# Masked attention and two gated layers on one core: six tiles per pair scaled on ScalarE, the split of q and k in eight operations of 384 columns, another order in the first unit of layer one

## The chip, the core and the metric

One core of one Trainium2 chip. Its engines are TensorE (PE, with its weight loads PEld), VectorE (DVE), ScalarE (ACT) and GpSimd (POOL); SyncE (SP) issues the transfers. Each engine takes its own instructions in order, and semaphores tie them together. The metric is the device time of one launch in microseconds, median of the runs.

## The reference

Everything is fp32. Attention over 2 x 8 heads, 768 positions and 64 dimensions, where a query sees only the keys with the same six-bit sign code:

```python
q_bits = (np.einsum('bhsd,dk->bhsk', q, proj) > 0)      # k alike
mask = q_bucket[:, :, :, None] == k_bucket[:, :, None, :]
scores = np.where(mask, scale * np.matmul(q, k.transpose(0, 1, 3, 2)), -1e9)
attn = np.exp(scores - np.max(scores, axis=-1, keepdims=True))
attn = attn / (np.sum(attn, axis=-1, keepdims=True) + 1e-09)
x = np.matmul(attn, v)                                  # heads side by side: 1536 x 512
x = (((x @ w1) * (x @ w2)) @ w3) @ w_out                # d_ff 1024
y = (1 / (1 + np.exp(-(x @ w_gate))) * (x @ w_val)) @ w_out2   # d_ff 1536
```

## The kernel before, in words

TensorE works on fp32r operands, so each fp32 operand is split in a rounded high part and a lower part (the difference), and a product is three matmuls (high x high, high x low, low x high). The splits are the work of the other engines: a rounding (a copy or an add of zero into an fp32r tile) and a subtraction.

**Attention.** Eight pairs of heads, `pair(p)` on each engine; PE runs pair 0, a loop over pairs 1 to 6, and pair 7. A pair has `STEPS` = 12 tiles of 128 queries, tiles 0 to 5 of the first head and 6 to 11 of the second. `UQ` = 3 tiles make a half of a head. For tile k the engines do, each in its own fixed order:

- PE (`pair`, L1271): at k = 1 the code bits of the next pair; `scores` of tile k+2 (four matmuls, L1197; they wait for the exp of tile k); a third of `values` of the half before (four matmuls, L1224); for k >= 4 one piece of `fill`, the product of w3 and w_out (three matmuls, L1257 to L1259); `transpose` of tile k (six, L1209). The transposes wait for the scaled tile (`norm_done`) and, bank by bank, for `pt_lo` of tile k-1.
- DVE (`pair`): `row_max` of tile k+1 (L924), `sum_eps`, `exp_scale`, `inverse` and `exp_bias` (four small ones; `sum_eps` and `inverse` are of tile k and wait for its exp, the other two are of tile k+1), `normalise` of tile k (L949, `prob` times `rnorm`, 128x768) unless ScalarE does it, then `transposed_lo` of tile k-1 (L957, two subtractions into `pt_lo`, each after its half of `pt_hi`), and `code` at k = 2.
- ACT (`pair`): at k = 0 a copy of the `fill` bank (`wp`); at k = 1, 4, 7, 10 the two copies of `attention_halves`; `transposed_hi` of tile k-1 (L617, two copies into `pt_hi`); the scaling of tile k where `k % UQ in NORM_ON_ACT` (L693; it waits for DVE's `rnorm`); then `exp` of tile k+1 (L650, with the sum along the row). Pair 0 also rounds wo1 after k = 3, 4, 6, 7; pair 6 (`ahead`) rounds the first weights of layer one after k = 8 and k = 9 (`pair_raw_high`, `pair_sums_high`); pair 7 (`last`) rounds a first-layer operand after each of k = 9, 10, 11 (`x_operand_high`).
- POOL (`pair`): `attention_sum(p, 0)`, which waits for ACT's halves at k = 1; `w3_split(1)`; `qk_split(p + 1)`, the high and lower part of the next pair's q and k, one instruction each over 1536 columns (L432 and L450, tile `hl`); `scale_q_codes`; `attention_sum(p, 1)`; `v_split` of one head (L432, L458, 384 columns each); `w3_split(0)`; `v_split` of the other head. In a middle pair the `qk_split` lies beside tiles 3 and 4. Pair 6 adds T3's sums and the first weight sums; pair 7 has no `qk_split`, but the sums T2 and T1 (`x_sum`, four of 768 columns), the split of B11 and the rounding of T3.
- SP: per pair two loads of w3 and v, the load of q and k of pair p+2 (after `hl_ready`), and `assemble` for each head, nine copies from `hl`, `codes` and `q_codes` into `sq` and `mk`. `assemble(0)` waits for `hl_ready`, `q_codes_done` and the scores of tile 5; PE's first scores of the next pair wait for it.

**Layer one** follows in units of seven products (a Strassen-like scheme over blocks of x: B11, T3, T2, T1, B22, B21, T4), each on two sides, six matmuls a side (L1296 to L1298). T3 is B22 less the block of pairs 0 and 1, T2 = T3 + B11, T1 = B22 - T2 and T4 = B21 - T2 are sums of blocks. PE's `unit(0, 0)` starts while attention ends: after B11 come the last three parts of `values`, then T3, T2, T1, B22, B21, T4. T2 waits for `u1_kept`, T1 for `u2_kept`, B22 for `u4_kept`: ScalarE's copies of the running bank (`kept1`, `kept2`, `kept4`), which stand in ACT's written-out order among the roundings `x_operand_high` of the operands. The lower parts `x_operand_low` are DVE's, in place over the raw block (L976), in the order `X_LOW_ORDER`. The lower part of T2 overwrites T2, which T4 = B21 - T2 still needs (`x_sum4`, L984), and B21 holds the output of pair 7; so T2's lower part on a side waits for `attention_out` (L963) of that side. B11's split and T3's rounding are POOL's, ahead of time. Then POOL makes the weight sums and lower parts of the next unit (`pair_weights`); PE's next unit waits for `g_ready`. Units run on to the end of layer one, then layer two and three in the same way.

## Time and profile before

| | us |
|---|---|
| median of 3 runs | 776.63 (776.06 to 777.81) |
| the profiled execution, its own time | 775.34 |
| its span | 773.3 |
| busy PE / PEld | 731.5 / 675.3 |
| busy DVE / ACT / POOL | 480.9 / 456.2 / 345.2 |
| granted TensorE clock, mean | 0.995 of full |

About 2.0 us of the profiled execution lie outside its span. Busy times are sums over an engine's instructions; an instruction that waits for something after it has started counts as busy for that time too. A timeline row has the start and length in us, engine, line, operation, what it writes and reads, the number of instructions merged in it, and in brackets the idle time before it with what ended it. A group row has the busy time of the group and the mean ns of one instruction. A middle pair lasts from 135.77 to 171.30 in the rows below, measured from `pt_lo` of tile 2 to the same of the next pair: in it tile 3's transposes are at 136.37, tile 4's at 140.13 and tile 10's at 157.21. The rows of tile 0 to tile 3 late in that window (161 to 171 us) belong to the next pair; what is at 170.06 there was at about 134.53 in the pair before.

### The profile page before, as it was taken

Reading aid. Unit: us, or ns where it says so; the run is one execution under the profiler, and the core shown is the slowest. Engines: PE = TensorE matmul, PEld = TensorE weight load, DVE = VectorE, ACT = ScalarE, POOL = GpSimd, SP = SyncE. Lnnn points to the kernel's source line nnn. Section 1 sums busy time; section 2 is a strip of 40 time slices with the busy share of each in tenths; the row PEclk is TensorE's granted clock in tenths of the full one; section 3 lists DMA queues with packets and bytes.
Section 4 is the critical chain, followed back from the end, with each engine's and each line's share of the span. In section 5 each row is a group of like instructions: output and inputs, shape, how many; then the busy total and the mean of one; then the engine's idle time right before and its main releaser. Section 6 shows DMA issues by size and latency. Waiting matters only on the chain.

```text
span 773.3 us, 12684 instructions
## 1 busy us (share of the span) xinstructions
PE 731.5 (95%) x4136; PEld 675.3 (87%) x4136; DVE 480.9 (62%) x1032; ACT 456.2 (59%) x842; POOL 345.2 (45%) x253
## 2 busy tenths in 40 slices
PE   6798989899898989799999999999999999999998
PEld 4687878778797878799999999999999999988886
DVE  5899999999999999832432833624324326774100
ACT  5788888897888988545446424564454454715100
POOL 3867364554628697164466600054653554140000
PEclk9999999999999999999999999999999999999999
DMA  5774443436273500001001000010010010401001
GB/s 154 219 175 105 116 124 94 129 89 165 71 175 91 115 12 18 28 28 56 28 27 54 1 0 1 1 55 28 28 54 28 27 55 0 163 1 68 28 28 41
DMA packets 26609, 51.79 MB, mean 67 GB/s; under 512 B 4161, under 2 KB 12689, under 8 KB 26577
## 3 DMA queue, kind: packets, MB, share of 16 engines
q1 hardware_dynamic: 26272, 51.32, 24.4%
q8 instruction: 17, 0.28, 0.1%
q14 instruction: 16, 0.12, 0.0%
q10 hardware_dynamic: 304, 0.07, 0.0%
HBM read 29.43 MB, written 3.15 MB: 42 GB/s over the span
## 4 chain that ended last, share of the span: by engine, by line
PE 74%; DVE 13%; issue 6%; ACT 4%; DMA 2%; SPq 1%; DVEq 0%; ACTq 0%
PE pair_bank L1296 14%; PE pair_bank L1298 14%; PE pair_bank L1297 13%; PE bank L1296 5%; PE bank L1298 5%; PE bank L1297 5%; PE bank L1224 5%; PE bank L1209 5%; PE pair_bank L1197 4%; DVE pt_lo L957 4%; DVE rowmax L924 4%; ACT pt_hi L617 2%; DMA qk_raw<-in_qk 2%; DVE prob L949 1%; PE bank L1258 1%
## 5 line engine op out<-in xcount | busy, mean ns | idle before, releaser
L1062 DVE TENSOR_TENSOR u<-bank,u 128x384 f32<-128x384 f32 x80 | 44.3, 555 | 135.5 <-ACT u L617 126.6
L617 ACT ACTIVATE u<-pair_bank 128x384 f32<-128x384 f32 x120 | 58.7, 491 | 109.3 <-PE pair_bank L1298 109.1
L1209 PEld LDWEIGHTS bank<-ident,prob 128*128 128x128 f32 x576 | 65.8, 141 | 49.7 <-DVE pt_lo L957 29.7
L1209 PE MATMUL bank<-ident,prob 128*128 128x128 f32 x576 | 85.3, 281 | 24.9 <-DVE pt_lo L957 24.3
L617 ACT ACTIVATE pt_hi<-bank 128x384 fp32r<-128x384 f32 x192 | 85.8, 489 | 32.2 <-PE bank L1209 31.7
L957 DVE TENSOR_TENSOR pt_lo<-bank,pt_hi 128x384 fp32r<-128x384 f32 x192 | 97.4, 548 | 7.8 <-ACT pt_hi L617 7.5
L650 ACT ACTIVATE prob<-pair_bank,ebias,escale 128x768 f32<-128x768 f32 x96 | 95.1, 991 | 7.2 <-DVE ebias L935 7.0
L924 DVE TENSOR_REDUCE rowmax<-pair_bank 128x1 f32<-128x768 f32 x96 | 90.9, 947 | 4.2 <-PE pair_bank L1197 4.0
L1197 PE MATMUL pair_bank<-mk,sq 128*128 128x384 f32 x384 | 89.7, 356 | 3.6 <-ACT prob L650 1.9
L1296 PE MATMUL pair_bank<-y_hi,g_hi 128*128 128x384 f32 x240 | 80.3, 335 | 0.0
L1197 PEld LDWEIGHTS pair_bank<-mk,sq 128*128 128x128 f32 x384 | 65.2, 191 | 8.8 <-issue 6.2
L491 POOL TENSOR_TENSOR g_sum<-g_raw,g_raw 128x256 f32<-128x256 f32 x20 | 17.9, 896 | 116.7 <-PE bank L1298 112.3
L504 POOL TENSOR_TENSOR g_raw_lo<-g_raw,g_hi 128x768 fp32r<-128x768 f32 x20 | 38.6, 1932 | 65.0 <-ACT g_hi L617 65.0
L1224 PE MATMUL bank<-pt_hi,v_st 128*128 128x384 f32 x192 | 67.2, 350 | 0.0
L1224 PE MATMUL bank<-pt_lo,v_st 128*128 128x384 f32 x192 | 64.6, 337 | 0.0
L949 DVE TENSOR_SCALAR prob<-prob,rnorm 128x768 f32<-128x768 f32 x64 | 59.8, 934 | 0.0
L1296 PE MATMUL pair_bank<-x_hi,g_hi 128*128 128x384 f32 x160 | 54.5, 340 | 3.0 <-DVE x_sum_lo L976 2.6
L509 POOL TENSOR_TENSOR g_sum_lo<-g_sum,g_hi 128x1024 fp32r<-128x1024 f32 x20 | 48.4, 2418 | 13.6 <-ACT g_hi L617 13.6
L1297 PE MATMUL pair_bank<-b_lo,g_hi 128*128 128x384 f32 x144 | 48.2, 335 | 0.0
L1298 PE MATMUL pair_bank<-y_hi,g_sum_lo 128*128 128x384 f32 x144 | 48.2, 335 | 0.0
L1296 PE MATMUL pair_bank<-wo_hi,gv_hi 128*128 128x512 f32 x120 | 46.8, 390 | 0.0
L1297 PE MATMUL pair_bank<-wo_lo,gv_hi 128*128 128x512 f32 x120 | 46.7, 390 | 0.0
(162 smaller groups left out, 1953.6 us busy)
## 6 DMA issues: line engine op xcount, KB each, us to landing
sq<-hl SPq DMA_DIRECT2D x45, 192.0 KB
mk<-hl SPq DMA_DIRECT2D x15, 384.0 KB
qk_raw<-in_qk SPq DMA_DIRECT2D x7, 768.0 KB, 5.6
w_raw<-in_w SPq DMA_DIRECT2D x16, 256.0 KB, 2.7
v_raw<-in_v SPq DMA_DIRECT2D x16, 192.0 KB, 2.7
wo_raw<-in_wo SPq DMA_DIRECT2D x12, 256.0 KB, 3.6
out<-out_sb SPq DMA_DIRECT2D x12, 256.0 KB, 2.0
mk<-hl SPq DMA_DIRECT2D x15, 192.0 KB
```

The source lines that it names most:

```text
L509: pool.tensor_tensor(g_sum_lo[j][:, :, :], g_sum[j][:, :, :], g_hi[j][:, S1:7, :].bitcast(F32), ALU.subtract).then_inc(g_ready, 1)
L617: return act.activation(dst, src, ACT.Copy)
L650: act.activation(prob[k % 3][:, :].rearrange("p (c n) -> p c n", c=KC), pair_bank[k % 2][:, :, 0:HALF], ACT.Exp, bias=ebias[:, k:k + 1], s ...
L924: dve.tensor_reduce(rowmax[:, k:k + 1], pair_bank[k % 2][:, :, 0:HALF], AX.XY, ALU.max).then_inc(max_done, 1)
L949: dve.tensor_scalar(prob[k % 3][:, :], prob[k % 3][:, :], rnorm[:, k:k + 1], None, ALU.mult).then_inc(norm_done[k % UQ], 1)
L957: dve.tensor_tensor(pt_lo[(k // UQ) % 2][cut], t_bank[j][:, 0:384].rearrange("p (t n) -> p t n", t=3), pt_hi[(k // UQ) % 2][cut].bitcast(F ...
L1197: mm = pe.matmul(pair_bank[k % 2][:, kc, 0:HALF], sq[hd][:, part, q0:q0 + 128], mk[hd][:, part, HALF * kc:HALF * kc + HALF], start=(part = ...
L1209: mm = pe.transpose(t_bank[j][:, 128 * t:128 * t + 128], prob[k % 3][:, 128 * (3 * j + t):128 * (3 * j + t) + 128], ident[:, :])
L1224: mm = pe.matmul(pv_bank[:, 0:HALF], v_st[hd][:, kt, :], moving[slot][:, kt, :], start=(kt == 0 and moving is pt_hi), stop=(kt == QT - 1 a ...
L1296: pe.matmul(dst, hi, m_hi, start=start, stop=False, skip_group_check=partial)
L1297: pe.matmul(dst, hi, m_lo, start=False, stop=False, skip_group_check=partial)
L1298: return pe.matmul(dst, lo, m_hi, start=False, stop=stop, skip_group_check=partial)
```

## The change

`NORM_ON_ACT` lists tiles of a pair now and not tiles of a half: ScalarE scales tiles 2, 3, 5, 8, 9 and 11 (before 2, 5, 8, 11), VectorE the other six. `qk_split` rounds q's two halves and k's two halves one by one, then subtracts in the same order, eight instructions of 384 columns; `hl_ready` counts four per pair, and SP waits for the last of them. In the first unit of layer one, B22's split is GpSimd's, behind T3's rounding. T4's sum is made in two parts: the half of the channels that pair 6 supplies at once (`x_sum4_begin`), while ScalarE keeps a copy of T2's other half (`x_take_t2`) from which `x_sum4` makes the rest once pair 7's output is there; so T2's lower part no longer waits for that output. The orders of ACT and DVE are written anew: B21's roundings stand ahead of `kept4`, T4's behind them.

```diff
@@ -53,7 +53,7 @@
 WARM = (10, 30)
-NORM_ON_ACT = (2,)
+NORM_ON_ACT = (2, 3, 5, 8, 9, 11)
@@ -67,9 +67,8 @@
 LOW_ORDER = (B11, T3, T1, B22, T2, B21, T4)
-X_HI_ORDER = ((T2, 0), (T2, 1), (T1, 0), (T1, 1), (B22, 0), (B21, 0), (B22, 1), (T4, 0), (B21, 1), (T4, 1))
-X_LOW_ORDER = ((T3, 0), (T3, 1), (T2, 0), (T1, 0), (T2, 1), (T1, 1), (B22, 0), (B22, 1), (B21, 0), (B21, 1),
-               (T4, 0), (T4, 1))
+X_HI_ORDER = ((T2, 0), (T2, 1), (T1, 0), (T1, 1), (B21, 0), (B21, 1), (T4, 0), (T4, 1))
+X_LOW_ORDER = ((T3, 0), (T3, 1), (T2, 0), (T2, 1), (T1, 0), (T1, 1), (B21, 0), (B21, 1), (T4, 0), (T4, 1))
 PAIRS1, PAIRS3 = KF // 2, KF2 // 2
@@ -244,6 +243,7 @@
         x_sums_done, x_sum4_done = sem("x_sums_done"), sem("x_sum4_done")
+        x_sum4_begun, x_t2_taken = sem("x_sum4_begun"), sem("x_t2_taken")
         x_hi_early, x_low_early = sem("x_hi_early"), sem("x_low_early")
@@ -355,9 +355,11 @@
+                if not isinstance(scored, int):
+                    sp.compute_val(4 * pairs - 3)
                 if hd == 1:
                     sp.wait_ge(s_done, scored)
-                sp.wait_ge(hl_ready, pairs)
+                sp.wait_ge(hl_ready, 4 * pairs - 3)
                 sp.wait_ge(q_codes_done, pairs)
@@ -370,7 +372,7 @@
                 if not last:
-                    load_qk(p + 2, p + 2, p + 2)
+                    load_qk(p + 2, 4 * p + 5, p + 2)
                 assemble(0, p + 2, STEPS * p + QT)
@@ -445,10 +447,13 @@
                 pool.wait_ge(assembled[1], copied(1, p - 1))
-                rounded(hl[:, 0::2, :], qk_raw[:, :, :]).then_inc(qk_hi_done, 1)
-                pool.wait_ge(qk_hi_done, p + 1)
-                pool.tensor_tensor(hl[:, 1::2, :], qk_raw[:, :, :], hl[:, 0::2, :].bitcast(F32),
-                                   ALU.subtract).then_inc(hl_ready, 1)
+                pieces = [(t, slice(HALF * hf, HALF * hf + HALF)) for t in range(2) for hf in range(2)]
+                for t, cols in pieces:
+                    rounded(one(hl[:, 2 * t, cols]), one(qk_raw[:, t, cols])).then_inc(qk_hi_done, 1)
+                for n, (t, cols) in enumerate(pieces):
+                    pool.wait_ge(qk_hi_done, 4 * p - 2 + n)
+                    pool.tensor_tensor(hl[:, 2 * t + 1, cols], qk_raw[:, t, cols], hl[:, 2 * t, cols].bitcast(F32),
+                                       ALU.subtract).then_inc(hl_ready, 1)
@@ -566,6 +571,14 @@
                         rounded(x_high(T3, side), x_raw(T3, side)).then_inc(x_hi_early, 1)
+                    pool.wait_ge(s_done, STEPS * PAIRS)
+                    for side in range(2):
+                        rounded(x_high(B22, side), x_raw(B22, side)).then_inc(x_hi_early, 1)
+                    for side in range(2):
+                        pool.wait_ge(x_hi_early, side + 5)
+                        pool.wait_ge(x_sums_done, side + 5)
+                        pool.tensor_tensor(x_low(B22, side), x_raw(B22, side), x_high(B22, side).bitcast(F32),
+                                           ALU.subtract).then_inc(x_low_early, 1)
                 if ahead:
@@ -630,7 +643,7 @@
-                if q in (T1, B22):
+                if q == T1:
                     act.wait_ge(s_done, STEPS * PAIRS)
@@ -639,8 +652,15 @@
                 if q == T4:
+                    act.wait_ge(x_sum4_begun, 1)
                     act.wait_ge(x_sum4_done, side + 1)
                 copy(x_high(q, side), x_raw(q, side)).then_inc(x_hi_done, 1)
+
+            def x_take_t2():
+
+                act.wait_ge(x_sums_done, 4)
+                act.wait_ge(wp_done, PAIRS)
+                copy(x_sums[T4][0][:, :, 1, :], x_sums[T2][0][:, :, 1, :]).then_inc(x_t2_taken, 1)
@@ -688,7 +708,7 @@
                         transposed_hi(p - 1, STEPS - 1)
-                    if k % UQ in NORM_ON_ACT:
+                    if k in NORM_ON_ACT:
                         act.wait_ge(rnorm_done, s + 1)
@@ -788,23 +808,22 @@
+            x_take_t2()
             kept1(0, 0, 0, u_x)
...
             kept1(0, 0, 1, u_x)
+            x_operand_high(T1, 1)
             attention_halves(3, PAIRS - 1, keep=False)
-            x_operand_high(T1, 1)
-            x_operand_high(B22, 0)
+            kept2(0, 0, 0, u_x)
             x_operand_high(B21, 0)
-            kept2(0, 0, 0, u_x)
-            x_operand_high(B22, 1)
             kept2(0, 0, 1, u_x)
+            x_operand_high(B21, 1)
             kept4(0, 0, 0, u_x)
+            kept4(0, 0, 1, u_x)
             x_operand_high(T4, 0)
-            kept4(0, 0, 1, u_x)
-            x_operand_high(B21, 1)
-            gate(ACT.Copy, 0, 0, y4_mm, 0, 0, y_bank[0], g12_done)
             x_operand_high(T4, 1)
-            gate(ACT.Copy, 0, 1, y4_mm, 0, 0, y_bank[1], g12_done)
+            for side in range(2):
+                gate(ACT.Copy, 0, side, y4_mm, 0, 0, y_bank[side], g12_done)
             pair_sums_high(1, 1)
@@ -969,19 +988,30 @@
                     dve.wait_ge(x_hi_done, X_HI_ORDER.index((q, side)) + 1)
-                if q in (T2, B21):
+                if q == T2:
+                    dve.wait_ge(x_sums_done, 5 + side)
+                    dve.wait_ge(x_sum4_begun, 1)
+                    dve.wait_ge(x_t2_taken, 1)
+                if q == B21:
+                    dve.wait_ge(x_sum4_begun, 1)
                     dve.wait_ge(x_sum4_done, side + 1)
-                if q in (T2, B22):
-                    dve.wait_ge(x_sums_done, 5 + side)
                 dve.tensor_tensor(x_low(q, side), x_raw(q, side), x_high(q, side).bitcast(F32),
...
+            def x_sum4_begin():
+
+                dve.wait_ge(x_done, 2 * (PAIRS - 1))
+                dve.wait_ge(x_sums_done, 4)
+                dve.wait_ge(wp_done, PAIRS)
+                dve.tensor_tensor(x_sums[T4][0][:, :, 0, :], x_f[:, PAIRS - 2, :].rearrange("p (s n) -> p s n", s=2),
+                                  x_sums[T2][0][:, :, 0, :], ALU.subtract).then_inc(x_sum4_begun, 1)
+
             def x_sum4(side):
+                late = x_sums[T4][0][:, side, 1, :]
                 dve.wait_ge(x_done, 2 * PAIRS - 1 + 2 * side)
-                dve.wait_ge(x_sums_done, 3 + side)
-                dve.wait_ge(wp_done, PAIRS)
-                dve.tensor_tensor(x_raw(T4, side), x_raw(B21, side), x_raw(T2, side),
+                dve.wait_ge(x_t2_taken, 1)
+                dve.tensor_tensor(late, x_f[:, PAIRS - 1, HALF * side:HALF * side + HALF], late,
                                   ALU.subtract).then_inc(x_sum4_done, 1)
@@ -1006,7 +1036,7 @@
                         exp_bias(*nxt)
-                    if k % UQ not in NORM_ON_ACT:
+                    if k not in NORM_ON_ACT:
                         normalise(p, k)
@@ -1042,18 +1072,20 @@
             transposed_lo(PAIRS - 1, STEPS - 1)
-            dve.wait_ge(x_done, 2 * (PAIRS - 1))
+            x_sum4_begin()
+            x_operand_low(T2, 0)
+            x_operand_low(T2, 1)
             dve.wait_ge(x_kept, 4 * PAIRS - 1)
...
             x_sum4(0)
-            x_operand_low(T2, 0)
             x_operand_low(T1, 0)
+            x_operand_low(T1, 1)
             attention_out(slice(0, D), 1, x_f[0:D, PAIRS - 1, HALF:SEQ])
...
             x_sum4(1)
-            for q, side in X_LOW_ORDER[4:10]:
-                x_operand_low(q, side)
+            x_operand_low(B21, 0)
+            x_operand_low(B21, 1)
@@ -1370,6 +1402,8 @@
                     pe.wait_ge(exp_done, STEPS * PAIRS - 1)
+                elif q == B22:
+                    pe.wait_ge(x_low_early, side + 3)
                 else:
```

## Rows read from the trace of the kernel before

**Rows 1.** Windows: us, PE, PEld, DVE, ACT, POOL busy (instructions), clock, DMA, GB/s
```profile
135.77:171.30 35.53, 32.75 (x200) 28.52 (x200) 34.56 (x94) 30.35 (x62) 17.88 (x14) 1.00 0.47 119
...
328.00:428.00 100.00, 99.63 (x575) 99.31 (x574) 36.21 (x67) 49.21 (x87) 55.71 (x44) 1.00 0.13 37
```

**Rows 2.** TensorE's timeline: transposes of tiles 3, 4 and 10 of a middle pair
```profile
136.37 1.01 PE L1209 MATMUL bank<-ident,prob 128*128 128x128 f32 x6 [1.02 <-DVE pt_lo L957]
...
140.13 1.01 PE L1209 MATMUL bank<-ident,prob 128*128 128x128 f32 x6 [1.34 <-DVE pt_lo L957]
...
157.21 1.01 PE L1209 MATMUL bank<-ident,prob 128*128 128x128 f32 x6 [0.19 <-DVE pt_lo L957]
```

**Rows 3.** VectorE's timeline: scaling of tiles 4, 9, 10, 3; T3's lower parts
```profile
138.00 1.61 DVE L949 TENSOR_SCALAR prob<-prob,rnorm 128x768 f32<-128x768 f32 x1
...
152.21 0.62 DVE L949 TENSOR_SCALAR prob<-prob,rnorm 128x768 f32<-128x768 f32 x1
...
155.34 1.34 DVE L949 TENSOR_SCALAR prob<-prob,rnorm 128x768 f32<-128x768 f32 x1
...
170.06 1.32 DVE L949 TENSOR_SCALAR prob<-prob,rnorm 128x768 f32<-128x768 f32 x1
...
301.93 2.36 DVE L976 TENSOR_TENSOR x_lo<-x_f,x_hi 128x768 fp32r<-128x768 f32 x2
```

**Rows 4.** GpSimd's timeline beside those scalings
```profile
135.51 3.68 POOL L450 TENSOR_TENSOR hl<-qk_raw,hl 128x1536 fp32r<-128x1536 f32 x1
...
155.25 1.01 POOL L458 TENSOR_TENSOR v_st<-v_raw,v_st 128x384 fp32r<-128x384 f32 x1
...
168.21 2.75 POOL L432 TENSOR_TENSOR hl<-qk_raw,zeros 128x1536 fp32r<-128x1536 f32 x1
```

**Rows 5.** GpSimd's groups by form in the middle pair, 384 columns
```profile
L458 POOL TENSOR_TENSOR v_st<-v_raw,v_st 128x384 fp32r<-128x384 f32 x2 | 2.0, 1014 | 0.2
...
L432 POOL TENSOR_TENSOR v_st<-v_raw,zeros 128x384 fp32r<-128x384 f32 x2 | 1.6, 824 | 3.0 <-PE bank L1224 3.0
```

**Rows 6.** ScalarE's timeline: tiles 5, 9, 10; 2, 4; last row pair 6
```profile
141.70 0.94 ACT L693 ACTIVATE prob<-prob,rnorm 128x768 f32<-128x768 f32 x1
...
153.34 1.00 ACT L650 ACTIVATE prob<-pair_bank,ebias,escale 128x768 f32<-128x768 f32 x1
...
169.15 0.87 ACT L617 ACTIVATE pt_hi<-bank 128x384 fp32r<-128x384 f32 x2
...
170.18 0.99 ACT L650 ACTIVATE prob<-pair_bank,ebias,escale 128x768 f32<-128x768 f32 x1 [0.16 <-DVE ebias L935]
...
171.28 0.48 ACT L617 ACTIVATE x_tmp<-bank 64x384 f32<-64x384 f32 x1
...
263.01 0.85 ACT L617 ACTIVATE pt_hi<-bank 128x384 fp32r<-128x384 f32 x2
```

**Rows 7.** TensorE's timeline: first product, T2, T1, T4, second unit
```profile
303.63 0.35 PE L1296 MATMUL pair_bank<-x_hi,g_hi 128*128 128x384 f32 x1
...
313.97 0.45 PE L1296 MATMUL pair_bank<-x_hi,g_hi 128*128 128x384 f32 x1 [2.65 <-DVE x_sum_lo L976]
...
316.20 0.52 PE L1297 MATMUL pair_bank<-x_sum_lo,g_hi 128*128 128x384 f32 x1
...
326.20 0.44 PE L1296 MATMUL bank<-x_hi,g_hi 128*128 128x384 f32 x1 [1.73 <-DVE x_sum_lo L976]
...
327.36 0.34 PE L1296 MATMUL pair_bank<-x_hi,g_hi 128*128 128x384 f32 x1
```

**Rows 8.** Window inside the first unit, columns of rows 1
```profile
316.00:318.00 2.00, 2.00 (x8) 2.00 (x7) 1.39 (x2) 0.92 (x2) 0.00 (x0) 0.50 0.00 0
```

**Rows 9.** GpSimd's timeline: B11's lower parts, T3's rounding, first sum
```profile
291.15 3.65 POOL L564 TENSOR_TENSOR x_lo<-x_f,x_hi 128x768 fp32r<-128x768 f32 x2
...
294.75 3.21 POOL L432 TENSOR_TENSOR x_hi<-x_f,zeros 128x768 fp32r<-128x768 f32 x2
...
302.41 1.07 POOL L491 TENSOR_TENSOR g_sum<-g_raw,g_raw 128x256 f32<-128x256 f32 x1 [4.45 <-PE bank L1259]
```

## The prediction

> **What bounds the kernel now.** I read the windows first. From 328 us on TensorE is busy 99.6 of 100 us [rows 1]: there the change touches nothing, so only what happens before the second unit of layer one counts. In a middle pair of heads the same row form gives TensorE 32.75 of 35.53 us, VectorE 34.56 and ScalarE 30.35 [rows 1]. So VectorE looks like the bound, with GpSimd half idle (17.88).
>
> Second, TensorE's timeline in that pair. Its waits stand ahead of the transposes of three tiles: 1.02 us at tile 3, 1.34 at tile 4, 0.19 at tile 10, each for pt_lo, which VectorE writes [rows 2]. Third, VectorE's own timeline: part of its busy time is waiting. Scaling a tile takes 0.62 us at tile 9, but 1.32 at tile 3, 1.61 at tile 4 and 1.34 at tile 10 [rows 3]. Each long one ends about 0.42 us after a GpSimd instruction ends: 168.21+2.75 is 170.96 and the scaling ends at 171.38; 135.51+3.68 is 139.19 against 139.61; 155.25+1.01 is 156.26 against 156.68 [rows 3, 4]. VectorE's scaling therefore waits for whichever GpSimd instruction is running, and then takes 0.42. The two instructions of 1536 columns that split q and k are the ones behind tiles 3 and 4.
>
> **Tiles 3 and 9 go to ScalarE** (tiles 2, 5, 8, 11 are there already). Two scalings leave VectorE, two of 0.94 [rows 6] join ScalarE: 30.35 plus 1.9 is 32.2 us a pair, still under the period that comes out. But the order inside the engines counts, so I walk the two places.
>
> Tile 3 and 4, in the trace's times. ScalarE ends pt_hi of tile 2 at about 170.0 (from 169.15 [rows 6]); the reciprocal is ready then; it scales tile 3 until 170.94 and the exp of tile 4, which was at 170.18, starts at 170.84 and ends with its sum at 171.9. VectorE, free of the scaling, starts pt_lo of tile 2 at 170.1 in place of 171.30, so the transposes of tile 3 can start at 171.0, where they started at 171.9 (136.37 a pair later [rows 2]). The row maximum of tile 5 follows at 171.1; the reciprocal of tile 4 waits for ScalarE's sum, and VectorE asks to scale tile 4 at 172.4 (before: 138.00, a pair later 173.53).
>
> **The split in eight pieces** decides how long that waits. A piece of 384 columns costs what v's split of 384 columns costs, 0.82 and 1.01 [rows 5]: 4 x 0.824 + 4 x 1.014 = 7.35 us, against 2.75 + 3.67 = 6.42. GpSimd pays 0.9 us more per pair and has 17 us free; q_codes, and SP's assembly copies behind it, move back by the 0.9, under a slack that I put at some 5 us, since the copies of a head are issued half a pair ahead of the scores that need them. That is costed at nothing; without that cover it is 0.9. The second half of the pieces runs from 171.5 to 175.5 with borders every 1.01 us. The scaling of tile 4 waits 0 to 1.0 for a border and ends at 172.95 to 173.95. pt_lo of tile 3 also needs pt_hi of tile 3, which ScalarE, after the two attention halves of 0.5 each [rows 6], has half ready at 173.44. So tile 4's transposes start at 174.05 to 174.5 in place of 175.66 (140.13 a pair later [rows 2]): a gain of 1.15 to 1.6, and I take 1.4. From there to tile 9 TensorE runs at its own pace before and after.
>
> Tile 9 and 10. ScalarE now scales tile 9 before exp of tile 10, which moves from 153.34 to 154.18 [rows 6]; two attention halves of 1.0 follow, and pt_hi of tile 9 starts at 156.2, half ready at 156.68. VectorE's pt_lo of tile 9 started at 156.6 before, held up by tile 10's scaling. So the 0.85 that ScalarE gets late takes the place of the 0.7 that VectorE stalled: gain 0 (bounds -0.2 and +0.2).
>
> Six pairs (1 to 6) have all this: 6 x 1.4 = 8.4 us. Pair 0 has the split too, but its ScalarE also splits wo1 at tiles 3 and 4: 0.5 (0 to 1.0). In pair 6 ScalarE has two splits of layer one's first weights between tiles 8 and 10 and has no gap there: pt_hi of tile 9 follows exp and the halves at once at 263.01 [rows 6], so its extra 0.85 comes through: -0.8. In pair 7 tile 4's scaling waits for GpSimd's sums of 768 columns, which stay whole; it asks for the port 0.3 us earlier, which mostly changes nothing: +0.3 (0 to 1.1). Also there, two operand splits precede tile 10, and ScalarE's extra 0.85, with the copy of T2 behind it, puts tile 11's transposes 1.1 late. Attention alone: 8.4 + 0.5 - 0.8 + 0.3 - 1.1 = 7.3 us.
>
> **The first unit.** Before, TensorE waits 2.65 us for T2's second side; a stretch at clock 0.50, the lower of its two levels (1.2 GHz), follows [rows 7, 8], where some ten matmuls take 0.52 for 0.33 with starts 0.15 further apart, 1.5 us; then 1.73 us for T4's second side, and the second unit starts at 327.36 [rows 7]. The edit makes T2's lower part independent of the last pair's output: that wait goes. What is late next? VectorE must make T3's lower parts before it reaches pt_lo of tile 11, and B22 on GpSimd is new beside it: two roundings of 1.6 and two subtractions of 1.83 [rows 9], from 297.5 (297.96 in [rows 9], less the port waits that tiles 3 and 9 no longer cause) to about 304.9. Two-input work of VectorE alternates with GpSimd, instruction by instruction: two T3 parts of 0.86 took 2.36 because one GpSimd sum of 0.74 came between, which itself showed 1.07 [rows 3, 9]. So T3's parts end at 307.3 (before 304.3), pt_lo of tile 11 at 308.25, and the values behind B11 wait 1.5 us: B11 starts at 304.7 (303.63 [rows 7] and 1.1) and takes 2.1, twelve matmuls at the 575 per 100 us of [rows 1]. The values and T3 then run to 312.5 (2.1 each); T2 waits 0.5 behind GpSimd's raw-weight part; T1 waits 0.75 (its lower part at 315.85, behind the attention output and the half sum); and B22 waits 1.05, because ScalarE's copy u4 stands behind B21's second rounding, which needs the last attention output. B21 and T4 follow without a wait and unit two starts at about 325.4, GpSimd's g_sum_lo for it being ready at 325.25. No wait is as long as the 2.65, so I count no stretch at the lower clock. Start against 327.36: 1.9 earlier, which includes the 1.1 late of pair 7. The unit itself is thus worth 3.0. Bounds: GpSimd's instructions always running first, and the clock falling once more, leave 0; VectorE always first, no waits but T1's, gives 5.5.
>
> **Sum.** 7.3 + 3.0 = 10.3 us. The profiled execution took 775.34 us, so 765.0; the median of the three runs is 776.63, 1.3 above it, so 766.3.
>
> **Rivals.**
> Border taken by GpSimd (slower). At a border the next piece is already queued behind the last. If it got the port ahead of the waiting VectorE, tile 4's scaling would wait for all eight, to 175.5, ending at 175.9; pt_lo and transposes follow at 176.5 against 175.66, +0.8 in each of six pairs, +4.8; with -0.8 of pair 6 and no gain in unit and pair 0: 776.63 + 5.6 = 782.2. It decides from the point where the pairs lose over 0.3 us each, since all other terms together give 1.9. Against it: in [rows 3, 4] tile 3's scaling gets in between the two long instructions, 0.42 after the first ends. For it only that no row shows eight in line. Chance 0.06.
> The Trainium skill, "SBUF — State Buffer", section "Who interferes with whom", says of the port pair that VectorE and GpSimd share that whoever issues first holds it for a whole instruction and the other is blocked. By that rule the queued piece could be the first, and the time would be this rival's; the pauses in this trace agree with the blocking, but show VectorE served at the border.
> ScalarE becomes the bound. If tile 10's late pt_hi isn't covered by the old stall, each pair loses 0.85 of its 1.4: 6 x 0.55 = 3.3, total 5.2, 771.4. For it: its load of 32.2 in 34.1 and its strict order. Against: the walk above. Chance 0.15.
> The unit gives nothing: its waits add up to what they replace, or a new long pause brings the lower clock. Total 7.3, 769.3. Chance 0.17.
> Moved work is hidden anyway: GpSimd's long instruction was only a coincidence of the tile 4 wait, and ScalarE's tiles cost what they free. Within 0.2% of 776.6. Chance 0.05.
> The forecast: 0.57.
>
> **Numbers.** 766.3. The forecast's own range is 762.5 to 769 (pairs 6.9 to 9.6, unit 1 to 5, pair 7 and the base 1 more); taking in the two middle rivals up to 771 leaves the slower one, the null and a little on each side out: 762 to 771. A difference under 0.2%, 1.6 us, is what a measurement can't tell from none. Faster by more: 0.88 (forecast, both middle rivals); within: 0.05; slower: 0.07 (the border rival and a little for order effects that I don't see).
>
> **What would show it.** Right: pair period 34.1 us (33.9 to 34.4); TensorE's wait at tile 3 under 0.4 and tile 4 under 0.8; tile 10's wait unchanged near 0.2 but after pt_hi on ScalarE; eight pieces of 0.8 and 1.0; 48 scalings on each engine, those of VectorE at most 1.6 long outside pair 7; no 2.65 wait at T2 but three or four of 0.5 to 1.5, at the values behind B11, T1 and B22; granted clock 1.0 around them. Wrong: a scaling on VectorE of several us beside the pieces (border rival); a period of 34.9 or more with pt_hi late at tiles 4 and 10 (ScalarE); from the first product to the second unit no less than the 23.7 us of before (327.36 less 303.63 [rows 7]), or a stretch at clock 0.5.

## The result and the profile after

The change makes the kernel faster: 768.51 us (median of 4 runs, 768.26 to 769.20) against 776.96 (4 runs, 776.06 to 777.81), a ratio of 0.9897 [0.9881, 0.9912], that is 8.4 us. Forecast were 10.3 us and 766.3. The profiled execution took 768.27 us, with a span of 766.5, against 775.34 before: 7.07 us less. The accounts below are made on that pair of executions.

The page of the kernel after, its engines, and VectorE's scalings as a group (form and count, busy and mean ns of one, idle before):

```profile
PE 734.3 (96%) x4136; PEld 674.1 (88%) x4136; DVE 466.5 (61%) x1015; ACT 467.5 (61%) x857; POOL 357.3 (47%) x299
...
L968 DVE TENSOR_SCALAR prob<-prob,rnorm 128x768 f32<-128x768 f32 x48 | 47.2, 983 | 0.0
```

VectorE has 48 scalings, ScalarE the other 48. VectorE's mean is 983 ns where one that meets nothing takes 0.62 us [rows 3], so waiting has not gone from them.

Windows of the kernel after, the columns of [rows 1], a middle pair, the first unit and a stretch that the change doesn't touch:

```profile
134.00:168.57 34.57, 33.22 (x201) 28.48 (x201) 33.06 (x92) 31.89 (x64) 18.51 (x20) 1.00 0.51 122
300.46:320.31 19.85, 17.48 (x98) 16.38 (x97) 18.42 (x23) 13.23 (x25) 9.71 (x6) 1.00 0.09 27
328.00:428.00 100.00, 98.99 (x570) 98.38 (x569) 43.02 (x71) 46.99 (x80) 54.63 (x41) 1.00 0.11 34
```

The pair fell from 35.53 to 34.57 us. The unit, from its first product to the next unit's, fell from 23.73 us (303.63 to 327.36 [rows 7]) to 19.85, all of it at a granted clock of 1.00. From there on nothing changed: TensorE is busy throughout.

The whole, measured by the start of tile 0's transposes in each pair, of tile 11's in the last, and of the second unit's first product (TensorE's timelines of both kernels):

| stretch | before | after | earlier by | forecast |
|---|---|---|---|---|
| launch to pair 0's tile 0 | 17.57 | 18.33 | -0.76 | 0 |
| pair 0 | 38.80 | 38.33 | 0.47 | 0.5 |
| pairs 1 to 5 | 177.60 | 172.84 | 4.76 | 7.0 |
| pair 6 | 35.87 | 36.60 | -0.73 | 0.6 |
| pair 7, tile 0 to 11 | 32.38 | 32.95 | -0.57 | -0.8 |
| tile 11 to the second unit | 25.14 | 21.26 | 3.88 | 3.0 |
| sum | 327.36 | 320.31 | 7.05 | 10.3 |

Two rows miss: the middle pairs give 0.95 each in place of 1.4 (a period of 34.57 us, outside the 33.9 to 34.4 that was to show the forecast right), and pair 6 loses. TensorE's timeline of the middle pair shows where (transposes of tiles 3, 4, 6, 7 and 10; the last bracket is the wait):

```profile
133.94 0.87 PE L1241 MATMUL bank<-ident,prob 128*128 128x128 f32 x6 [0.18 <-DVE pt_lo L976]
137.15 1.01 PE L1241 MATMUL bank<-ident,prob 128*128 128x128 f32 x6 [0.58 <-DVE pt_lo L976]
...
143.55 0.82 PE L1241 MATMUL bank<-ident,prob 128*128 128x128 f32 x6
145.79 1.01 PE L1241 MATMUL bank<-ident,prob 128*128 128x128 f32 x6
...
154.67 1.01 PE L1241 MATMUL bank<-ident,prob 128*128 128x128 f32 x6 [0.27 <-DVE pt_lo L976]
```

The waits of 1.02 and 1.34 at tiles 3 and 4 [rows 2] are now 0.18 and 0.58. From tile 0 (125.80) to tile 4 are 11.35 us, before (127.40 to 140.13) 12.73: the forecast 1.4 is there, 1.38. It is spent again at tile 7. From tile 6 to 7 there are 2.24 us where there were 2.07 (146.53 to 148.60), and from 7 to 8 3.63 for 3.45, since tile 7's transposes, held up halfway, take 1.01 where they took 0.82; with 0.08 at tile 10 that makes the loss of 0.43.

VectorE's timeline, the scalings of tiles 4 and 6:

```profile
135.21 1.43 DVE L968 TENSOR_SCALAR prob<-prob,rnorm 128x768 f32<-128x768 f32 x1
...
141.06 1.45 DVE L968 TENSOR_SCALAR prob<-prob,rnorm 128x768 f32<-128x768 f32 x1
```

and GpSimd's, the eight pieces and the split of v:

```profile
131.09 3.19 POOL L434 TENSOR_TENSOR hl<-qk_raw,zeros 128x384 fp32r<-128x384 f32 x4
134.23 4.22 POOL L455 TENSOR_TENSOR hl<-qk_raw,hl 128x384 fp32r<-128x384 f32 x4
...
140.17 0.83 POOL L434 TENSOR_TENSOR v_st<-v_raw,zeros 128x384 fp32r<-128x384 f32 x1
141.08 1.01 POOL L463 TENSOR_TENSOR v_st<-v_raw,v_st 128x384 fp32r<-128x384 f32 x1
```

Tile 6's scaling starts by the trace just as v's subtraction begins (141.06 and 141.08), and it is the scaling that waits. The subtraction ends at 142.09; the scaling ends at 142.51, again 0.42 later. In the kernel before the two did not meet, by GpSimd's and VectorE's timelines:

```profile
142.12 1.02 POOL L458 TENSOR_TENSOR v_st<-v_raw,v_st 128x384 fp32r<-128x384 f32 x1
```
```profile
144.03 0.62 DVE L949 TENSOR_SCALAR prob<-prob,rnorm 128x768 f32<-128x768 f32 x1
```

Counted from the pair's tile 0, v's subtraction stood at 14.72 us and the scaling at 16.63. After, the subtraction stands at 15.28 and the scaling at 15.26, earlier by what was gained. GpSimd's split of q and k ends 0.86 later (12.65 for 11.79 from tile 0); 0.3 of that comes back in `q_codes`, which takes 0.83 us where it took 1.14, and v's subtraction is 0.56 later.

In pair 6 one longer instruction is behind v's. TensorE's waits at tiles 7 and 10:

```profile
250.56 1.01 PE L1241 MATMUL bank<-ident,prob 128*128 128x128 f32 x6 [1.20 <-DVE pt_lo L976]
...
260.39 1.01 PE L1241 MATMUL bank<-ident,prob 128*128 128x128 f32 x6 [1.21 <-DVE pt_lo L976]
```

T3's two sums on GpSimd, and tile 7's scaling on VectorE beside the second of them:

```profile
245.64 3.98 POOL L557 TENSOR_TENSOR x_f<-x_f 128x768 f32<-128x768 f32 x2
```
```profile
248.25 1.78 DVE L968 TENSOR_SCALAR prob<-prob,rnorm 128x768 f32<-128x768 f32 x1
```

The scaling ends at 250.03, 0.41 after the sums (249.62), and TensorE waits 1.20 where before it waited for nothing. The 1.21 at tile 10 is the loss behind ScalarE that was forecast as 0.8; it measured 0.82 (3.43 us from tile 9 to 10, before 2.61).

The first unit: its first product, the attention values behind B11, T1, B22 and the second unit:

```profile
300.46 0.33 PE L1328 MATMUL pair_bank<-x_hi,g_hi 128*128 128x384 f32 x1
...
303.62 0.45 PE L1256 MATMUL bank<-pt_hi,v_st 128*128 128x384 f32 x1 [0.92 <-DVE pt_lo L976]
...
310.64 0.44 PE L1328 MATMUL pair_bank<-x_hi,g_hi 128*128 128x384 f32 x1 [0.50 <-DVE x_sum_lo L998]
...
313.97 0.41 PE L1328 MATMUL pair_bank<-x_hi,g_hi 128*128 128x384 f32 x1 [0.95 <-ACT u L630]
...
320.31 0.44 PE L1328 MATMUL pair_bank<-x_hi,g_hi 128*128 128x384 f32 x1
```

The waits of 2.65 and 1.73 [rows 7] and the stretch at the lower clock [rows 8] are gone. Three of the four waits that were forecast to take their place are there.

### The profile page after: what moved, and what is told of

It reads as the page before. It is cut to its first block, busy times and chain, and to the rows that moved or that the text cites. A ratio compares the mean times of both kernels' runs of the same rounds, so it can differ in the third digit from the quotient of the medians.

```text
span 766.5 us, 12753 instructions
## 1 busy us (share of the span) xinstructions
PE 734.3 (96%) x4136; PEld 674.1 (88%) x4136; DVE 466.5 (61%) x1015; ACT 467.5 (61%) x857; POOL 357.3 (47%) x299
## 4 chain that ended last, share of the span: by engine, by line
PE 75%; DVE 9%; ACT 7%; issue 6%; DMA 1%; SPq 0%; ACTq 0%; DVEq 0%
PE pair_bank L1328 14%; PE pair_bank L1329 14%; PE pair_bank L1330 14%; PE bank L1329 6%; PE bank L1328 6%; PE bank L1330 5%; PE bank L1241 5%; PE bank L1256 5%; PE pair_bank L1229 4%; DVE pt_lo L976 3%; DVE rowmax L943 2%; ACT prob L670 2%; ACT pt_hi L630 2%; DMA qk_raw<-in_qk 1%; PE bank L1290 1%
## 5 line engine op out<-in xcount | busy, mean ns | idle before, releaser
L509 POOL TENSOR_TENSOR g_raw_lo<-g_raw,g_hi 128x768 fp32r<-128x768 f32 x20 | 38.7, 1934 | 65.2 <-ACT g_hi L630 65.2
L968 DVE TENSOR_SCALAR prob<-prob,rnorm 128x768 f32<-128x768 f32 x48 | 47.2, 983 | 0.0
L1330 PE MATMUL pair_bank<-wo_hi,gv_lo 128*128 128x512 f32 x120 | 46.7, 389 | 0.0
```

Source lines behind the costliest of these rows:

```text
L968: dve.tensor_scalar(prob[k % 3][:, :], prob[k % 3][:, :], rnorm[:, k:k + 1], None, ALU.mult).then_inc(norm_done[k % UQ], 1)
L1330: return pe.matmul(dst, lo, m_hi, start=False, stop=stop, skip_group_check=partial)
```

## The experiments

Two theories went in. A: what a GpSimd instruction costs is the rest of it that a VectorE scaling must sit out, so the gain depends on which piece each scaling meets. B: scaling moved to ScalarE brings the gain by VectorE's load, and the pieces matter little. The totals scatter by pair 0 (below), so the periods from the traces are the finer measure. "pair" is the period of a middle pair, "unit" the time from tile 11's transposes to the second unit:

| kernel | us (range, runs) | ratio to before | pair | pair 6 | pair 7 | unit |
|---|---|---|---|---|---|---|
| e1_norm_only | 781.18 (777.14-784.53, 12) | 1.0053 [1.0030, 1.0076] | 35.4, 37.0 | 38.68 | 32.97 | 23.64 |
| e2_split_only | 773.99 (772.35-775.32, 12) | 0.9952 [0.9931, 0.9972] | 34.81 | 36.04 | 32.44 | 25.13 |
| e3_reorder_only | 774.45 (772.50-775.38, 12) | 0.9963 [0.9944, 0.9983] | 35.52 | 35.90 | 32.40 | 22.25 |
| e6_without_tile9 | 769.44 (768.35-771.55, 6) | 0.9901 [0.9866, 0.9936] | 34.49 | 35.75 | 32.12 | 22.26 |
| g1_norm_undone | 771.23 (770.94-772.38, 5) | 0.9925 [0.9898, 0.9952] | 34.81 | 36.07 | 32.41 | 22.27 |
| g2_tile6_for_9 | 769.44 (768.18-770.36, 4) | 0.9898 [0.9864, 0.9932] | 34.73 | 35.43 | 33.11 | 21.00 |
| g3_sums_in_halves | 768.22 (767.52-768.90, 4) | 0.9881 [0.9849, 0.9914] | 34.57 | 35.87 | 32.09 | 22.36 |
| g4_sixteen_pieces | 769.71 (769.58-770.52, 4) | 0.9903 [0.9871, 0.9935] | 34.63 | 35.79 | 32.91 | 21.30 |
| g5_kept4_first | 768.28 (767.77-769.36, 4) | 0.9894 [0.9866, 0.9923] | 34.56 | 36.56 | 32.96 | 20.89 |
| h1_rounding_whole | 766.27 (765.70-767.05, 4) | 0.9874 [0.9845, 0.9902] | 34.24 | 36.26 | 32.94 | 21.27 |
| h2_kept4_raw_pieces | 767.67 (767.17-769.90, 4) | 0.9896 [0.9865, 0.9926] | 34.57 | 36.56 | 32.93 | 20.72 |
| h4_combined | 765.38 (763.87-768.05, 6) | 0.9865 [0.9838, 0.9891] | 34.16 | 34.72 | 32.13 | 21.82 |

### The scaling alone, on the kernel before

```diff
-NORM_ON_ACT = (2,)
+NORM_ON_ACT = (2, 3, 5, 8, 9, 11)
...
-                    if k % UQ in NORM_ON_ACT:
+                    if k in NORM_ON_ACT:
...
```

> Only tiles 3 and 9 go to ScalarE; the split stays two long instructions and the first unit keeps its old order. Theory A (VectorE's scaling waits for the end of whichever GpSimd instruction is running): tile 4's scaling still waits for the same long instruction, so its transposes do not move, the pair period stays at 35.3 to 35.6 us and the extra ScalarE work in pairs 6 and 7 costs 0.7 each: total 0 to 2 us slower than before. Theory B (what pays is VectorE's work being taken away): period about 34.6, total 5 us faster than before.

By itself this part makes the kernel slower, by 4.1 us (0.53% of 777.27). VectorE's scaling of tile 4, GpSimd's subtraction of 1536 columns, and TensorE's wait in its trace:

```profile
137.44 2.60 DVE L949 TENSOR_SCALAR prob<-prob,rnorm 128x768 f32<-128x768 f32 x1
```
```profile
136.15 3.47 POOL L450 TENSOR_TENSOR hl<-qk_raw,hl 128x1536 fp32r<-128x1536 f32 x1
```
```profile
140.56 1.05 PE L1209 MATMUL bank<-ident,prob 128*128 128x128 f32 x6 [1.75 <-DVE pt_lo L957]
```

VectorE comes to tile 4 earlier and so sits out more of the same instruction: 136.15 plus 3.47 is 139.62, the scaling ends at 140.04. Of the 0.83 us that tile 3 gives (8.15 us from tile 0, before 8.98), tile 4 leaves 0.20 (12.53, before 12.73). In three of the pairs (3, 4 and 6) a stretch at the lower clock follows that wait, and the periods of pairs 3 and 4 are 36.93 and 37.00 where their neighbours have 35.4. A's period of 35.3 to 35.6 came in the pairs without such a stretch; its total, 0 to 2 us slower, did not: three stretches at the lower clock, some 1.5 us each, account for the excess. B wanted a period of 34.6 and falls.

### The split alone, on the kernel before

```diff
-                rounded(hl[:, 0::2, :], qk_raw[:, :, :]).then_inc(qk_hi_done, 1)
...
+                pieces = [(t, slice(HALF * hf, HALF * hf + HALF)) for t in range(2) for hf in range(2)]
+                for t, cols in pieces:
+                    rounded(one(hl[:, 2 * t, cols]), one(qk_raw[:, t, cols])).then_inc(qk_hi_done, 1)
```

with the subtractions and the counts of `hl_ready` as in the change.

> Only the split in eight pieces. Theory A: tile 3's scaling waits for a piece of 0.8 and not for 2.75, tile 4's at most 1.0: tile 3 gains 0.4, tile 4 0.9, period 34.6 to 35.1, total 3 to 5 us faster than before. Theory B: GpSimd only gets 0.9 us more work per pair, VectorE none less: period 35.5, total within 1 us of before.

Each pair falls by 0.71 us, inside A's expectation. The scalings of tiles 3 and 4 take 0.99 and 0.89 us, before 1.32 and 1.61 [rows 3]. The same trace already has the meeting at tile 6, v's subtraction at 144.68 and the scaling at 144.66 with 1.45 us. In e1, which has ScalarE's tiles without the pieces, tile 6 to 7 takes 2.06 us and 7 to 8 3.46, as before. So the pieces bring the meeting, not ScalarE's tiles.

### The reorder alone, and tiles 3 and 9 taken back

e3 is the changed kernel with both other parts undone; g1 undoes the scaling alone: `NORM_ON_ACT = (2, 5, 8, 11)`.

> Only the first unit's new order. If the terms are independent: pairs as before (35.5), and from the first product to the second unit about 20 us in place of 23.7, total 3 to 4.5 us faster than before. Rival, the unit gains only because attention before it has changed: less than 2 us.

> The changed kernel with ScalarE back at tiles 2, 5, 8, 11: split and first unit stay new. Theory A (waits for the running GpSimd instruction are what counts): pairs as with the split alone, 34.8 us, so tile 3's move is worth 0.25 a pair on top of the split, and the total is 1 to 3 us above the changed kernel's 768.5 (pair period +1.2 over five pairs; pairs 6 and 7 0.7 each the other way). Theory B (the moved scalings carry the gain): 5 us or more above.

e3 leaves the pairs alone and shortens the unit by 2.89 us (25.14 to 22.25); the total falls by 2.9 (0.37% of the kernel before), just under the 3 to 4.5 expected. In g1 the pair is 34.81: on top of the pieces the moves of tiles 3 and 9 are worth 0.24 a pair (tile 3's alone 0.32, as e6 below has 34.49), and the medians differ by 2.7 us (771.23 and 768.51). The periods explain 1.1 of these: 1.2 in five pairs and 1.0 in the unit, less 0.5 each in pairs 6 and 7; the rest is not placed. The totals of the parts don't add: alone they are worth -4.1, 3.7 (0.48%) and 2.9, together 2.5, and the whole, by its ratio too, gives 8.0. The scaling needs the pieces in so far as its long wait at tile 4, and the lower clock behind it, go only with them.

### Without tile 9

```diff
-NORM_ON_ACT = (2, 3, 5, 8, 9, 11)
+NORM_ON_ACT = (2, 3, 5, 8, 11)
```

> The changed kernel with tile 9 back on VectorE (ScalarE scales 2, 3, 5, 8, 11). Theory A with the walk of the prediction: in middle pairs nothing (34.4 to 34.7, against 34.57 of the changed kernel), in pairs 6 and 7 the 0.7 to 0.8 us that ScalarE was late come back: 1 to 2 us faster than the changed kernel, 766.5 to 767.5. Theory B: one more tile on VectorE costs about 0.5 per pair, 3 us or more slower than the changed kernel.

The periods came as expected: 0.08 a pair, 0.85 in pair 6, 0.83 in pair 7. The total did not. TensorE's timeline of this kernel in the first unit:

```profile
303.07 0.45 PE L1256 MATMUL bank<-pt_hi,v_st 128*128 128x384 f32 x1 [1.36 <-DVE pt_lo L976]
...
310.64 0.44 PE L1328 MATMUL pair_bank<-x_hi,g_hi 128*128 128x384 f32 x1 [1.05 <-DVE x_sum_lo L998]
```

Tile 11 comes 0.99 us earlier (298.06), yet T1 starts at 310.64, the same as in the changed kernel. The 0.99 has become waiting, 0.44 more behind B11 and 0.55 more at T1. GpSimd's part of pair 7 starts by its own queue, at 283.79 against 283.97 in the changed kernel, so it came only 0.18 earlier, and VectorE's T3 parts then take 4.31 us beside it where they took 3.87. GpSimd's lower part of the raw weights (L509) even starts later, at 306.15 against 305.28, and VectorE's half sum for the attention output meets it:

```profile
306.15 2.56 POOL L509 TENSOR_TENSOR g_raw_lo<-g_raw,g_hi 128x768 fp32r<-128x768 f32 x1
```
```profile
306.93 2.20 DVE L982 TENSOR_TENSOR x_f<-x_f,x_tmp 128x384 f32<-128x384 f32 x1
```

306.15 plus 2.56 is 308.71, and the half sum ends at 309.13, again 0.42 later. In the changed kernel it takes 0.55 and ends at 309.13 too, since there T2's lower parts met that instruction (3.73 us, here 2.62). T1's lower part starts at 309.64 here and at 309.63 there.

### Tile 6 for tile 9

```diff
-NORM_ON_ACT = (2, 3, 5, 8, 9, 11)
+NORM_ON_ACT = (2, 3, 5, 6, 8, 11)
```

> The changed kernel with tile 6 on ScalarE in place of tile 9 (2, 3, 5, 6, 8, 11). In the trace of the changed kernel VectorE's scaling of tile 6 takes 1.45 us beside GpSimd's split of v. Theory A: that stall goes, tile 10's old one comes back, the 0.35 us that tiles 7 and 8 start late is regained in part, since ScalarE's two attention halves of tile 7 now come 0.85 later: period 34.1 to 34.5; pair 6 gains 1 us (no wait for the sum of 768 columns at tile 6). Total 1 to 4 us under 768.5. Theory B (only the number of tiles on each engine counts): 34.57, within 0.5.

A miss. The collision at tile 6 is gone, but the period is 34.73, longer by 0.16: ScalarE now has the scaling, an exp and two attention halves (143.28 to 146.21) ahead of pt_hi, for which VectorE's pt_lo waits 0.39, and tile 7's transposes wait 0.28 behind it. ScalarE's load has a price of its own at this place. Where the partner was the long sum, in pair 6, the same edit does gain, 36.60 to 35.43.

### The long sums in halves

```diff
-                        pool.tensor_tensor(x_raw(T3, side), x_raw(B22, side), x_raw(T3, side),
-                                           ALU.subtract).then_inc(x_sums_done, 1)
+                        for t in range(2):
+                            half = pool.tensor_tensor(one(x_raw(T3, side)[:, t, :]), one(x_raw(B22, side)[:, t, :]),
+                                                      one(x_raw(T3, side)[:, t, :]), ALU.subtract)
+                        half.then_inc(x_sums_done, 1)
```

and pair 7's sums in the same way.

> The changed kernel with GpSimd's sums of 768 columns for T3 (pair 6), T2 and T1 (pair 7) in halves of 384. Theory A: VectorE's scalings of tiles 6 and 7 in pair 6 (1.45 and 1.78 us) and tile 4 in pair 7 (1.94) wait a piece of 1.0 at most: tile 7's transposes of pair 6 and tile 4's of pair 7 wait under 0.6 in place of 1.20 and 1.26, 1 to 1.5 us faster in all. Rival (those two waits are set by ScalarE's pt_hi): nothing. The middle pairs stay at 34.57.

Pair 6 falls from 36.60 to 35.87 (tile 7's wait from 1.20 to 0.49) and pair 7 from 32.95 to 32.09 (tile 4's from 1.26 to 0.72). So the size of these sums was their price, though tile 4's wait stayed above the 0.6 expected. And again the second unit starts almost where it did, 320.15: the unit grows by 1.1 us, with the same meeting as in e6 (L509 at 305.99, the half sum 2.19 us long), and the total is 0.3 us less in place of 1 to 1.5, a miss.

### Sixteen pieces

```diff
-                pieces = [(t, slice(HALF * hf, HALF * hf + HALF)) for t in range(2) for hf in range(2)]
+                pieces = [(t, slice(192 * hf, 192 * hf + 192)) for t in range(2) for hf in range(4)]
```

> The changed kernel with q's and k's split in sixteen instructions of 192 columns. Theory A with its bound, a wait ends at the first border: tile 4's scaling takes 0.45 to 1.0 us in place of 1.43, its transposes come up to 0.4 earlier (ScalarE's pt_hi of tile 3 then sets them), period 34.2 to 34.5, while GpSimd's split grows to about 8.5 us. If GpSimd could take the port first at a border, more borders are more chances and tile 4's scaling takes 2 us or more.

VectorE's scalings of tiles 4 and 6, then GpSimd's subtractions, its sum and the rounding of v:

```profile
137.15 0.62 DVE L968 TENSOR_SCALAR prob<-prob,rnorm 128x768 f32<-128x768 f32 x1
...
142.81 1.72 DVE L968 TENSOR_SCALAR prob<-prob,rnorm 128x768 f32<-128x768 f32 x1
```
```profile
136.76 4.81 POOL L455 TENSOR_TENSOR hl<-qk_raw,hl 128x192 fp32r<-128x192 f32 x8
...
142.31 1.01 POOL L469 TENSOR_TENSOR x_f<-x_f,x_tmp 128x384 f32 x1
143.28 0.82 POOL L434 TENSOR_TENSOR v_st<-v_raw,zeros 128x384 fp32r<-128x384 f32 x1
```

With eight subtractions in line, tile 4's scaling gets in at the first border, ahead of the queued piece. But the pair is 34.63, not the 34.2 to 34.5 expected: the pieces last longer together (4.81 for 4.22), GpSimd's queue comes later still, and tile 6's scaling takes 1.72, with a wait of 0.28 at tile 7. And here GpSimd does take a border: the scaling has waited since 142.81 when the sum ends at 143.32, v's rounding goes ahead of it until 144.10, and the scaling ends at 144.53. Served at the first border it would have ended at 143.74. All six looped pairs show this. The rival in which GpSimd takes the border is thus not disproved as a mechanism: it did not act at tile 4, and it does at tile 6 of this kernel. What decides who is served is open. Smaller pieces help only where they are met.

### The rounding whole, the subtraction in four

```diff
-                for t, cols in pieces:
-                    rounded(one(hl[:, 2 * t, cols]), one(qk_raw[:, t, cols])).then_inc(qk_hi_done, 1)
-                for n, (t, cols) in enumerate(pieces):
-                    pool.wait_ge(qk_hi_done, 4 * p - 2 + n)
+                rounded(hl[:, 0::2, :], qk_raw[:, :, :]).then_inc(qk_hi_done, 1)
+                pool.wait_ge(qk_hi_done, p + 1)
+                for t, cols in pieces:
```

> The changed kernel with the rounding of q and k as one instruction of 1536 columns again; only the subtraction stays in four pieces. With tiles 2 and 3 on ScalarE no scaling of VectorE falls beside the rounding. Theory A: GpSimd reaches the subtractions, and after them v's split, 0.4 us earlier, so tile 4's scaling (1.43) meets an earlier border and tile 6's (1.45) ends 0.4 earlier: period 34.1 to 34.4 in place of 34.57, total 1 to 2.5 us under 768.5. Rival (short instructions are better wherever they stand): period 34.6 or more.

GpSimd's timeline and VectorE's of this kernel:

```profile
129.88 2.74 POOL L434 TENSOR_TENSOR hl<-qk_raw,zeros 128x1536 fp32r<-128x1536 f32 x1
132.70 4.21 POOL L454 TENSOR_TENSOR hl<-qk_raw,hl 128x384 fp32r<-128x384 f32 x4
```
```profile
133.98 1.10 DVE L967 TENSOR_SCALAR prob<-prob,rnorm 128x768 f32<-128x768 f32 x1
...
139.63 1.31 DVE L967 TENSOR_SCALAR prob<-prob,rnorm 128x768 f32<-128x768 f32 x1
```

This is the clearest test of A. With tile 3 on ScalarE no scaling meets the rounding any more, and whole it costs 2.74 us where its four pieces cost 3.19. GpSimd is ahead by the difference, the scaling of tile 4 takes 1.10 for 1.43 and that of tile 6 1.31 for 1.45, and the pair falls by 0.33 to 34.24: 0.20 of it from tile 0 to 4 (11.15 us for 11.35), 0.15 from tile 6 to 7 (2.09 for 2.24). The ratio is 0.9874 against the changed kernel's 0.9897, with intervals that overlap; the five equal periods carry the verdict.

### Two edits in the first unit

g5 puts the copy of `kept4` ahead of `x_operand_high(B21, 1)` on ScalarE; h2 adds to it that the raw weights' lower part (L509) is made in three pieces of 256 columns.

```diff
             kept2(0, 0, 1, u_x)
-            x_operand_high(B21, 1)
             kept4(0, 0, 0, u_x)
+            x_operand_high(B21, 1)
             kept4(0, 0, 1, u_x)
```

> The changed kernel with ScalarE's copy u4 of the first side ahead of B21's second rounding. Walk of the prediction: B22 waits 0.95 us only because that copy stands behind a rounding that needs the last attention output. Then B22 starts right behind T1, 0.8 to 0.95 us earlier, and the second unit with it. Rival (B21's or T4's lower part is next in line): B22 earlier, but a wait of the same length at B21 or T4.

> As the one before, and GpSimd's lower part of the second unit's raw weights in three pieces of 256 columns. T2's second lower part waited for that long instruction (two T2 parts took 3.73 us). Theory A: it now waits a piece, T1's lower part comes about 1 us earlier and T1's wait of 0.50 goes: first product to second unit 18.2 to 18.8 us in place of 19.85. Rival (T1 waits for the attention output or for u2): as the one before.

In g5 B22's wait of 0.95 is gone. A new one stands where the second unit begins, on TensorE:

```profile
321.48 0.44 PE L1328 MATMUL pair_bank<-x_hi,g_hi 128*128 128x384 f32 x1 [0.52 <-POOL g_sum_lo L514]
```

From the first product to the second unit g5 takes 19.48 us for 19.85, so of 0.95 only 0.37 is kept, where 0.8 or more was expected. In h2 it takes 19.31, against 18.2 to 18.8 expected, a miss. VectorE, behind the pieces:

```profile
304.95 2.62 DVE L1004 TENSOR_TENSOR x_sum_lo<-x_sum,x_hi 128x768 fp32r<-128x768 f32 x2 [0.20 <-ACT x_hi L636]
307.50 1.09 DVE L988 TENSOR_TENSOR x_f<-x_f,x_tmp 128x384 f32<-128x384 f32 x1
308.62 0.98 DVE L1020 TENSOR_TENSOR x_sum<-x_f,x_sum 128x384 f32<-128x384 f32 x1
```

T2's lower parts fall from 3.73 to 2.62, but the next two operations, 0.55 and 0.56 in the changed kernel, now meet the later pieces and take 1.09 and 0.98. T1's wait goes only from 0.50 to 0.36.

### All that helped, together

h1, g3, h2's two edits, and tile 9 back on VectorE.

> All that Theory A asks for: tile 9 back on VectorE, rounding of q and k whole, the sums of pairs 6 and 7 in halves, u4's copy first and raw weights in pieces. Pairs 34.0 to 34.4, pair 6 34.8 to 35.2, first product to second unit under 20: total 764 to 766.5, about 3 us faster than the changed kernel and 1.4% under before. Rival (the waits only move to other tiles, and GpSimd's chain into the first unit holds its end where it is): 767.5 or more.

TensorE's waits in its first unit, at T1, inside B22 and at the second unit:

```profile
307.18 0.44 PE L1338 MATMUL pair_bank<-x_hi,g_hi 128*128 128x384 f32 x1 [1.30 <-DVE x_sum_lo L1008]
...
311.58 0.41 PE L1338 MATMUL pair_bank<-x_hi,g_hi 128*128 128x384 f32 x1 [0.62 <-ACT u L640]
...
317.55 0.44 PE L1338 MATMUL pair_bank<-x_hi,g_hi 128*128 128x384 f32 x1 [0.53 <-POOL g_sum_lo L513]
```

765.38 us, a ratio of 0.9865 [0.9838, 0.9891], where the changed kernel has 0.9897 [0.9881, 0.9912]: it beats the kernel before, and in all likelihood the changed one too. The pair is 34.16 and pair 6 34.72. Of what the attention brings, the unit takes back 0.6 (20.47 us from the first product, for 19.85 and the expected 20 at most), most of it at T1.

## Why the prediction was right, and where its steps were off

The likeliest case came out, the time of 768.51 lies in the forecast's own range of 762.5 to 769, and no rival's mechanism decided. But it lies there by 0.5 us and with luck: the six looped pairs gave 4.9 us before ScalarE's loss in pair 6, not 8.4 and below the 6.9 put as their lower bound, and the unit's 0.9 too much made up for part of it. With a unit of 3.0, as forecast, the time would have been about 769.4. Step by step:

- **VectorE's scaling waits out the GpSimd instruction that is running, then takes 0.42 us.** Right in each trace: 0.42 after v's subtraction, 0.41 after T3's second sum, 0.42 in e1 after the instruction of 1536 columns. The Trainium skill, "SBUF — State Buffer", section "Who interferes with whom", has the shared ports as an exclusive lock: the waits in the traces agree with it.
- **Border taken by GpSimd (the rival of 0.06).** Not in the changed kernel: there each of the 16 borders that a scaling met after waiting 0.2 us or more went to VectorE. But it exists: in g4 at tile 6 of each looped pair, and in the first pair of g4 and g5 (last section).
- **Tiles 3 and 4: 1.4 us a pair.** Right, 1.38 from tile 0 to tile 4. The pieces alone give 1.05 there (11.68 us for 12.73) and 0.71 in the whole pair, the scaling alone 0.20 there and 0.1 in the pair, or a loss where the lower clock follows.
- **"From there to tile 9 TensorE runs at its own pace before and after."** Wrong, and this is the step that failed. The walk moved VectorE by the 1.4 and GpSimd by the 0.9, and asked of neither what they now meet; tile 6's scaling meets v's subtraction, 0.35 us a pair, 1.8 in five pairs. The 0.9 was costed at nothing because SP's copies had slack. That cover held in the looped pairs (not in the first pair of g5, where TensorE waits 1.73 us for those copies); what the delay moved was the rest of GpSimd's own queue, under VectorE's scalings. h1, with 0.45 less delay, gets 0.15 back from tile 6 to 7, and 0.20 more at tile 4; the other 0.18, from tile 7 to 8, stays.
- **Tile 9 and 10: 0 (bounds 0.2).** It costs 0.08 a pair (e6).
- **Pair 6: -0.8 and the 1.4.** The ScalarE term measured 0.82 and the gain at tile 4 1.35 (12.61 to 11.26 us from tile 0). Missing was the same collision with a longer partner: tile 6 to tile 7 grew by 1.26 (2.16 to 3.42), T3's sums of 768 columns being next in GpSimd's queue. g3 halves them and gets 0.73 back.
- **Pair 7: +0.3 and -1.1.** 0.27 (tile 0 to 4 took 12.04, then 11.77) and -0.84 (tile 4 to 11, 20.34 and 21.18); e6 puts ScalarE's part at 0.83.
- **The first unit: 3.0, with waits of 1.5, 0.5, 0.75 and 1.05.** It gave 3.88. The waits were 0.92, none at T2, 0.50 and 0.95: in the right places with the right releasers, except T2's. VectorE's T3 parts took 3.87 us beside GpSimd, and were done 2.2 us after the first product, where the walk had 2.6. That no stretch at the lower clock would follow was right.
- **ScalarE becomes the bound.** Not in the changed kernel, where the pair holds 31.89 us of ScalarE's time in 34.57 and its share at tile 10 is 0.08. It shows at single places: tile 10 in pair 6, and tile 6 once it is moved there (g2).

What the sum had too much is thus 2.2 in the middle pairs and 1.3 in pair 6, against 0.9 too little in the unit and 0.2 in pair 7, and the launch took 0.76 longer: 10.3 - 2.2 - 1.3 + 0.9 + 0.2 - 0.8 is 7.1, the profiled difference. The medians differ by 8.4 and not 7.07 because the profiled execution of the kernel before lies 1.62 under its median, and that of the changed kernel 0.24 under its own.

Open: e6 and g3 turn 1.0 to 1.3 us of attention time into waiting in the unit. The place is shown (T1 and the values behind B11), and so is what VectorE meets there (GpSimd's queue starting at its old time, and its instruction L509), but a kernel in which GpSimd's part of pair 7 starts earlier was not tried. Open too is what decides a border between the two engines.

## What to carry to other kernels

Where VectorE and GpSimd both work in SBUF, read a GpSimd instruction's price not from its own duration but from which VectorE operation arrives while it runs, and whether that operation is of a kind that waits: cut it only where one does, and leave it whole where none does, since each cut delays the rest of GpSimd's queue. A border mostly lets VectorE in, but g4 shows that one can't count on it. When an edit shifts the two queues against each other, walk them on to the end of the period and into the stage behind; a gain on one and a delay on the other add up in what meets next. And test parts together as well as alone: a part that loses by itself (the scaling, 4.1 us) can gain beside another (0.24 us a pair on top of the pieces).
